# A leaner start of the first batch, its work in a new order, and the last output tile in two column halves

## The reference, cut to what matters

```
scores = q @ k.T / 8;  scores = where(mask, scores, -1e9)
attn = exp(scores - max) / sum;  out = attn @ v
```

## Time and profile before

| | us |
|---|---|
| median of 3 runs (718.87 to 719.3) | 718.95 |
| the profiled execution, its own time | 713.36 |
| its span, first to last instruction | 711.6 |
| PE busy | 700.3 (98%) |
| DVE busy | 303.6 (43%) |
| ACT busy | 288.3 (41%) |
| POOL busy | 97.4 (14%) |

### The profile page before, as it was taken

The page is one execution under the profiler, slowest core; times in us unless marked ns, Lnnn a source line. Parts: engine busy times, 40 slices in busy tenths (PEclk is TensorE's granted clock), DMA queues, the critical chain, the costliest instruction groups (busy, mean ns, idle before and its releaser), DMA issues.

```text
span 711.6 us, 15586 instructions
## 1 busy us (share of the span) xinstructions
PE 700.3 (98%) x5239; PEld 518.4 (73%) x5240; DVE 303.6 (43%) x916; ACT 288.3 (41%) x865; POOL 97.4 (14%) x138
## 2 busy tenths in 40 slices
PE   8999999999999999999999999999999999999997
PEld 8888777687676877776666777777676767777774
DVE  3854887158861788416657311112111211122111
ACT  3853778257872677614620223222322232222320
POOL 3310001000100001000022121112111221112113
PEclk9999999999999999999999999999999999999999
DMA  8783127330372213300026135611440770001101
GB/s 180 168 209 80 35 60 199 102 67 2 94 201 66 68 23 101 111 7 1 31 79 240 31 106 206 221 67 40 143 157 29 265 283 29 29 30 39 43 29 38
DMA packets 86467, 69.59 MB, mean 98 GB/s; under 512 B 69102, under 2 KB 69118, under 8 KB 86416
## 3 DMA queue, kind: packets, MB, share of 16 engines
q1 hardware_dynamic: 78816, 44.73, 22.5%
q0 software_dynamic: 7600, 24.19, 10.0%
HBM read 118.12 MB, written 11.27 MB: 182 GB/s over the span
## 4 chain that ended last, share of the span: by engine, by line
PE 96%; DVE 2%; ACT 1%; issue 1%; POOL 0%; ACTq 0%; DVEq 0%; POOLq 0%
PE bank L1314 22%; PE bank L1325 21%; PE bank L812 9%; PE bank L808 5%; PE bank L903 5%; PE bank L733 5%; PE bank L862 4%; PE bank L891 4%; PE bank L773 4%; PE bank L711 3%; PE bank L833 3%; PE bank L746 2%; PE bank L704 2%; PE bank L1297 1%; PE bank L700 1%; PE bank L838 1%
## 5 line engine op out<-in xcount | busy, mean ns | idle before, releaser
L1314 PEld LDWEIGHTS bank<-pt,stage_b 128*128 128x128 f32 x1344 | 155.0, 192 | 10.0 <-issue 10.0
L1325 PE MATMUL bank<-w_all,raw_all 128*128 x352 | 158.2, 593 | 0.0
L1314 PE MATMUL bank<-pt,stage_b 128*128 128x128 f32 x1344 | 156.9, 275 | 0.0
L1789 ACT ACTIVATE raw_all<-bank 128x512 f32<-128x512 f32 x44 | 26.3, 597 | 214.3 <-PE bank L1314 214.3
L1325 PEld LDWEIGHTS bank<-w_all,raw_all 128*128 128x128 f32 x352 | 63.6, 191 | 63.6 <-issue 63.6
L2388 DVE TENSOR_SCALAR raw_all<-bank,p_slot 128x512 f32 x21 | 15.8, 751 | 208.9 <-PE bank L1325 208.9
L625 POOL DMA_INDIRECT out_dram<-raw_all,idx_out x25 | 37.7, 1506 | 246.7 <-DVE raw_all L2388 229.8
L812 PE MATMUL bank<-stage_b,w_all 128*128 128x288 f32 x256 | 69.0, 415 | 0.6 <-issue 0.6
L1505 ACT ACTIVATE pr<-sm,negmax_a 96x80 f32<-96x80 f32 (+1 forms) x168 | 59.8, 359 | 3.2 <-DVE negmax_a L1841 3.1
L812 PEld LDWEIGHTS bank<-stage_b,w_all 128*128 128x128 f32 x256 | 46.3, 190 | 16.3 <-issue 5.2
L1494 ACT COPY w_sb<-bank 128x256 f32<-128x256 f32 (+5 forms) x93 | 37.6, 421 | 27.3 <-PE bank L862 25.9
(11 more groups left out here) (231 smaller groups left out, 902.4 us busy)
## 6 DMA issues: line engine op xcount, KB each, us to landing
w_sb<-in_moe_w_dram SPq DMA_DIRECT2D x19, 2048.0 KB
w_all<-in_moe_w_dram SPq DMA_DIRECT2D x19, 2048.0 KB
w_sb<-in_moe_w_dram POOLq DMA_DIRECT2D x12, 512.0 KB, 4.8
w_all<-in_moe_w_dram POOLq DMA_DIRECT2D x12, 512.0 KB, 4.7
mixture_rows<-y_sb SPq DMA_DIRECT2D x16, 256.0 KB, 2.1
raw_all<-in_q_dram SPq DMA_DIRECT2D x28, 144.0 KB
raw_all<-in_k_dram SPq DMA_DIRECT2D x28, 144.0 KB
v_dil<-in_v_dram SPq DMA_DIRECT2D x42, 80.0 KB, 3.4
```

The lines of the kernel that those rows point to most:

```text
L1314: last = pe.matmul(ps[half][:, f * P:(f + 1) * P], w1_sb[:, 0, c * F + at:c * F + at + P] if buf is None else w1_fix[:, c, at:at + P], xT[ ...
L1325: last = pe.matmul(ps[5], hidT[:, half * HALF + n * P:half * HALF + (n + 1) * P], w2_sb[:, bass.ds(buf, 1), half, n * D:(n + 1) * D].rearr ...
```

## The change

- TensorE runs 11 `turn_over` products before the first use, in place of 12, the band's product and 12. The band's product and its copy move behind uses 0 and 1.
- Inside the first stage the calls are put in a new order on TensorE, ScalarE and VectorE. The `turn_over` products there are 1 and 2 in the first part, and 1, 1, 3, 2, 1, 3, 3 toward the end (17 in all). The 8 router products stand one at a time between other calls, where they stood in one row before, and `pe_router_turn` stands much earlier, behind probabilities 2.
- SP issues `wo`, `w_gate2` and `w_local` before v of pairs 2 and 3.
- The fifth output tile is computed as two column halves: columns 0 to 255 go to partitions 0 to 63 of the bank and columns 256 to 511 to partitions 64 to 127. So `pe_out` has 4 products of 256 columns in place of 2 of 512, `move_y` copies 128 x 256 in place of 64 x 512, and `store_y` makes two transfers of 64 KB.

```diff
+        STORES = [2 + P // TILE[NT - 1], 2]
         def store_y(sp, b, t):
             n = TILE[t]
+            w = D * n // P
             sp.wait_ge(y_moved[t % 2], b * CNT2[t % 2] + t // 2 + 1)
-            sp.dma_start(xs[bass.ds(b * S + T0[t], n), :], y_sb[t % 2][0:n, :]).then_inc(y_stored[t % 2], 16)
+            for r in range(0, P, n):
+                c0 = r // n * w
+                sp.dma_start(xs[bass.ds(b * S + T0[t], n), c0:c0 + w], y_sb[t % 2][r:r + n, 0:w]
+                             ).then_inc(y_stored[t % 2], 16)
...
             load_qk(sp, 0, 3)
-            load_v(sp, 0, 2)
-            load_v(sp, 0, 3)
             sp.dma_start(wo_sb, ...)
             sp.dma_start(wr_sb[:, :, 0:EF], ...)
             sp.dma_start(wr_sb[:, :, EF:EF + 1], ...)
+            load_v(sp, 0, 2)
+            load_v(sp, 0, 3)
...
+            n = D * nq // P
             for p in range(PAIR_E):
-                last = pe.matmul(X[0:nq, :], OT[:, p, T0[t]:T0[t] + nq], wo_sb[:, p, :],
-                                 start=(p == 0), stop=(p == PAIR_E - 1))
+                for r in range(0, P, nq):
+                    c0 = r // nq * n
+                    last = pe.matmul(X[r:r + nq, 0:n], OT[:, p, T0[t]:T0[t] + nq], wo_sb[:, p, c0:c0 + n],
+                                     start=(p == 0), stop=(p == PAIR_E - 1))
...
         def _(pe):
             pe.wait_ge(ident_ready, 1)
-            turn_over(pe, S2[0], 12)
-            pe.wait_ge(band_top, 1)
-            pe.matmul(SA[QP:2 * QP, 0:(1 + NB) * KP], ...).then_inc(band_turned, 1)
-            turn_over(pe, S2[0], 12)
+            turn_over(pe, S2[0], 11)
             pe_first(pe, 0)
...
         def move_y(copy, eng, m, t):
-            copy(y_sb[t % 2][0:nq, :], X[0:nq, :]).then_inc(y_moved[t % 2], 1)
+            copy(y_sb[t % 2][:, 0:n], X[:, 0:n]).then_inc(y_moved[t % 2], 1)
```

## The result

| | before | after |
|---|---|---|
| median of 4 runs each | 719.12 us (718.87 to 719.37) | 709.27 us (707.61 to 709.6) |
| the profiled execution | 713.36 | 707.61 |
| its span | 711.6 | 705.9 |

The ratio of the means is 0.9858, with a 95% interval of 0.9841 to 0.9875; the medians stand 9.9 us apart. The forecast was 712.0 with a range from 709.8 to 716.5. The two profiled executions differ by 5.75 us only. So the medians hold some 4 us that the two first traces don't show.

The account below looks back on a forecast made before the run. TensorE's own list of work was taken to bound the kernel (96% of the chain of waits). First stage 3.5 us and fifth tile 4 x 0.88 = 3.5 us, off 718.95, gave 712.0 us, range 709.8 to 716.5.

Parts of the forecast that it names:

- The step that failed: Whole kernel: the timed median would stay 5.6 us above the profiled execution after the change.
- the sum (7.0): Whole kernel: total gain, 3.5 us from the first stage and 3.5 us from the fifth output tile.
- The clock rival: First stage: small uses may not keep TensorE at 2.4 GHz, making it slower, 730 through half the list; chance 0.05.
- The opening: Before the first use: 11 constants in place of 24, use 0 at 6.48 us, scores 0 at 11.0.
- The data: Opening loads: pair 0's q and k land before 6.48 us, pair 1 at about 7.5, so no cost.
- The first stage: From the opening to the first projection: 3.5 us gained, bounds 1.8 and 4.4.
- The waits at probabilities 11 and 12: Late first stage: TensorE waits for VectorE, then ScalarE, 0.2 us each; 0.9 us allowed with the close places.
- The wait for the gates: Before the router turn: gate loads landing 3 us later would stop TensorE 1.7 us, total 713.7; chance 0.06.
- the 0.20 for it: First stage: chance that ScalarE takes over as the bound, total gain about 5.5 us, time 713.5.
- The tile: Fifth output tile, four times: column halves take 0.98 us in place of 1.86, 3.5 us saved in all.
- the two estimates 0.94 and 1.02: Fifth output tile's cost in us: from halves streaming the same columns, and from each half streaming its own.
- The fourth tile: Fifth output tile's appearance in the routing: the full 0.88 us comes through, constants ending just as VectorE's scan does.

Follow-up runs that it names:

- row_kept: Kernel before, with only the constants (turn_over) behind the row of router products placed as 2, 3, 2, 4 in place of 3, 2, 6: 713.85 us, ratio 0.9951.
- fewer_open: gates_first with 7 opening constants in place of 11: 718.45 us, ratio 0.9999.
- opening_tail: Kernel before with the changes of opening_only and row_kept together: 712.56 us, ratio 0.9936.
- opening_tail_tile: opening_tail with the fifth output tile also as column halves: 707.71 us, ratio 0.9847.
- before_again: Kernel before, unchanged, run again in 10 executions: median 719.06 us.
- gates_first: Kernel after, with wo, w_gate2 and w_local issued before q and k of pair 3: 706.05 us, ratio 0.9829.
- first_only: Kernel after, but with the fifth output tile computed as before: 710.84 us, ratio 0.9896.
- tile_only: Kernel before, with only the fifth output tile as two column halves: 712.64 us, ratio 0.9929.
- after_again: Kernel after, unchanged, run again: 707.94 us, ratio 0.9863.
- spread_only: Kernel before, with router products one at a time around values 9 to 12 and constants 2, 3, 2, 4: 713.14 us, ratio 0.9933.
- opening_only: Kernel before, with 11 opening constants in place of 24 and the band's product and copy behind uses 0 and 1: 716.07 us, ratio 0.9956.
- row_router: Kernel after, with all eight router products in one row behind probabilities 10: 710.07 us, ratio 0.9869.

## Why the prediction was wrong, point by point

**The step that failed** is "The median of the runs stands 5.6 above the profiled one; I take that distance as kept". That number was for the most part a loss of clock that belonged to the kernel: 65 of 79 executions of before have a clock below 0.998, and the one traced runs 10.2 us at half pace at the end of the first stage and 3.4 us in the routing. Measured against 719.12, the distance was 5.8 us before the change, and after it it is 709.27 - 707.61 = 1.7. These 4.1 us are why the time came out below the range, although the two profiled executions differ by less (5.75) than the sum (7.0). What exactly makes the clock fall in before stays open; the runs show that it does, where, and that two constants placed elsewhere mostly end it. The distance was the largest unexplained number on the table. It called for a term of its own, or at least for a range that reached down to 718.95 - 7.0 - 5.6 = 706.3.

**The clock rival** was put on the wrong side only. The prediction asked whether the change could lose the clock, said "only the opening of this trace is slow", and did not ask whether the kernel before loses it in the executions that were timed. What the new order brought beyond the sum is that no execution falls below a clock of 0.995; in quiet ones it brought nothing that can be told, and row_kept gets most of the former by moving two constants. The warning itself was sound: fewer_open paid it.

**The opening**: use 0 at 6.62 and scores 0 at 11.15, forecast 6.5 and 11. The data were priced at nothing. That held in this trace but by less than I thought: behind 11 constants TensorE waited 0.16, 0.27 and 0.78 us for pair 0's k in three other traces. Counting bytes gave 5 us, and where the wait shows the landing it was at 6.1 to 6.6. Pair 1, counted as there at 7.5, made use 4 wait in opening_tail and opening_tail_tile, until 10.0 and 9.7. And the moment at which the pace doubles isn't fixed: the first 12 constants take 5.29 us in before, 4.37 in before_again and 5.42 in row_kept. The forecast took it from one trace.

**The first stage** gave 2.95, forecast 3.5. The waits at probabilities 11 and 12 did not come. The wait for the gates did, which was a rival at 0.06: SP issued the local gate at 17.6, not at 16.8, as issuing pair 3's q took 2.5 us in place of 1.5, and it took 6.0 us to land, not 4.9. In gates_first the first projection comes 0.97 earlier again, 3.9 in all. So ScalarE was no bound, and the 0.20 for it was too much.

**The tile**: 1.01 us, between the two estimates 0.94 and 1.02 and close to the one with each half streaming its own columns. Gain 3.4, forecast 3.5. The Trainium skill's rule that changing the tiling mode drains the array (TensorEngine Tiling (Array Packing), Key Properties) cost no more here than was forecast: 1.01 is 0.08 above half of the 1.86 before. The fourth tile came through in full, as worked out from the scan.

**Not foreseen**: 0.6 us at the copy behind the 40 small products. It also appears in first_only, tile_only and before_again (1.9 us in place of 1.29) and not in after_again, gates_first or row_kept. So it comes and goes between executions of one kernel and is not the change's.

## What to carry to other kernels

When the timed runs and the profiled one differ by more than the runs among themselves, explain that number before building on it: profile again and read the granted clock in stretches, not as one mean. Filler work is worth what it keeps up: two products moved 3.5 us ahead were worth 4.7 us at the median here, and four products left out cost 12. Cut fillers last, time many executions of each count, and put loads that a step needs early enough that no wait can open in a thin stretch: one of 2 us stood ahead of a loss of 20 us here.

## What the runs showed of the hardware

- TensorE's records stay gapless while its clock is halved: the busy share was 98% in quiet and lossy executions alike, and only durations and PEclk tell.
- A loss in the first stage lasted 3.4 us in opening_tail, 6.8 in spread_only, 10.2 in before_again and opening_only, and 20.5 after a late load (row_router) and after the short opening (fewer_open), though TensorE's records show it at work almost without a gap. The Trainium skill, TensorE: Matmul & The Clock Gate, What's actually happening, says that activity releases the throttle; here being busy by the records was not enough, and in before_again full pace came back only behind the six wide constants that start at 49.0.
- PEclk read 1.00 in the opening while the constants ran at 0.44 us each and then 0.24: the column does not show the slow start. In fewer_open seven executions of 716.8 to 719.6 us have a mean of 0.997 to 1.000, above the 0.985 of the three at 714.5.
- Products on the two column halves of the array overlap almost fully at 256 columns, with different moving data: 8 records in 1.01 us, where four of 512 columns on one half took 1.86.
